# Constant-operand products on TensorE during the pooled attention, and last stores issued from two queues

## The reference, cut to what matters

```python
q_d = q.reshape(B, H, Sd, factor, D).mean(axis=3)      # factor = 4, Sd = 144; k_d, v_d likewise
out_up = np.repeat(sm_attn(q_d, k_d, v_d), factor, axis=2)
mask = np.abs(pos[:, None] - pos[None, :]) < factor
scores = np.where(mask, scale * np.matmul(q, k.transpose(0, 1, 3, 2)), -1000000000.0)
...                                                    # softmax, times v: out_local
x = out_up + out_local                                 # then (B * S, H * D)
xn = x / rms * rms_g;  g = xn @ w_gate;  silu = g * (1.0 / (1.0 + np.exp(-g)))
y = silu * (xn @ w_val) @ w_out
h = y @ w_in;  r = np.maximum(h, 0.0);  return (s * (r * r) + b) @ w_out2
```

## Time and profile before

| what | value |
|---|---|
| median of 3 runs | 991.49 us (990.32 to 991.92) |
| the profiled execution's own time | 987.57 us |
| its span, first to last instruction | 985.8 us |
| PE busy | 947.4 us, 96% |
| DVE busy | 547.3 us, 56% |
| ACT busy | 355.0 us, 36% |
| POOL busy | 372.5 us, 38% |

### The profile page before, as it was taken

One profiled execution on the slowest core, in us unless ns is written; L12 is line 12 of the kernel. 1 busy time (PEld: TensorE's weight loads), 2 busy tenths in 40 slices (PEclk: granted clock), 3 DMA queues, 4 the chain that ended last, 5 costly groups with the idle time before them and its releaser, 6 DMA issues.

```text
span 985.8 us, 12910 instructions
## 1 busy us (share of the span) xinstructions
PE 947.4 (96%) x4836; PEld 771.7 (78%) x4864; DVE 547.3 (56%) x818; ACT 355.0 (36%) x816; POOL 372.5 (38%) x192
## 2 busy tenths in 40 slices
PE   5698899999999999999999999999999999999997
PEld 4687799766777777777778998888888888888896
DVE  6899997875774765564542324434433443343343
ACT  3348854762324222422241444222222322222232
POOL 5757776777783876455600454000000000000000
PEclk9999999999999999999999999999999999999999
DMA  9797664433331231012003332102001100100010
GB/s 251 210 257 240 179 189 134 124 111 105 93 112 38 83 107 46 16 37 69 19 2 127 130 128 64 43 1 86 1 1 43 43 1 1 65 1 1 1 43 23
DMA packets 54379, 79.41 MB, mean 81 GB/s; under 512 B 9836, under 2 KB 37068, under 8 KB 52908
## 3 DMA queue, kind: packets, MB, share of 16 engines
q1 hardware_dynamic: 52444, 71.79, 24.6%
q10 hardware_dynamic: 1872, 6.78, 1.8%
HBM read 67.05 MB, written 11.50 MB: 80 GB/s over the span
## 4 chain that ended last, share of the span: by engine, by line
PE 82%; DVE 7%; DMA 4%; issue 2%; ACT 2%; SPq 1%; POOL 1%; DVEq 0%; ACTq 0%; POOLq 0%
PE bank L779 26%; PE bank L919 7%; PE bank L920 7%; PE bank L921 7%; PE bank L903 7%; PE bank L901 7%; PE bank L902 7%; PE bank L815 5%; PE bank L813 5%; PE bank L814 5%; DMA rawq<-in_q_dram 1%; DVE sc L594 1%; DMA rawv<-in_v_dram 1%; DVE x L604 1%; ACT prod_a L576 1%
## 5 line engine op out<-in xcount | busy, mean ns | idle before, releaser
L549 POOL TENSOR_TENSOR prod<-qs,ks 128x896 f32<-128x896 f32 x80 | 179.4, 2264 | 85.8 <-DVE sc L594 68.8
L563 POOL TENSOR_TENSOR prod<-sc,vs 128x896 f32<-128x896 f32 x72 | 138.1, 2020 | 65.5 <-DVE x L604 31.3
L940 DVE SCALAR_TENSOR_TENSOR r<-bank,r 128x512 f32<-128x512 f32 (+1 forms) x80 | 51.1, 638 | 181.0 <-ACT r L928 181.0
L903 PE MATMUL bank<-y_h,w2i_l 128*128 128x512 f32 (+1 forms) x320 | 117.7, 368 | 0.0
L928 ACT ACTIVATE r<-bank 128x512 f32<-128x512 f32 (+1 forms) x80 | 44.4, 555 | 181.9 <-PE bank L903 181.2
L835 DVE TENSOR_TENSOR bank<-bank,u 128x512 f32<-128x512 f32 (+1 forms) x66 | 39.5, 599 | 116.9 <-PE bank L779 116.3
L813 PE MATMUL bank<-h_h,wo_h 128*128 128x512 f32 (+1 forms) x264 | 102.7, 389 | 0.0
L779 PE MATMUL bank<-x_h,wv_h 128*128 128x512 f32 (+1 forms) x264 | 100.4, 392 | 0.0
L594 DVE TENSOR_REDUCE sc<-prod 128x14 f32<-128x896 f32 x80 | 85.7, 1077 | 17.0 <-POOL prod L549 16.9
L815 PE MATMUL bank<-h_h,wo_l 128*128 128x512 f32 (+1 forms) x264 | 93.3, 353 | 0.0
L814 PE MATMUL bank<-h_l,wo_h 128*128 128x512 f32 (+1 forms) x264 | 92.5, 350 | 0.0
(11 more groups left out here) (135 smaller groups left out, 1941.1 us busy)
## 6 DMA issues: line engine op xcount, KB each, us to landing
raww<-in_moe_w_out_dram SPq DMA_DIRECT2D x14, 512.0 KB, 4.3
ks<-in_k_dram SPq DMA_DIRECT2D x16, 280.0 KB
vs<-in_v_dram SPq DMA_DIRECT2D x16, 280.0 KB, 4.3
y_scr<-y_st ACTq DMA_DIRECT2D x4, 1024.0 KB, 4.1
raww<-in_moe_w_in_dram SPq DMA_DIRECT2D x8, 512.0 KB, 3.8
y_raw<-y_scr SPq DMA_DIRECT2D x4, 1024.0 KB, 4.8
out_dram<-o_st SPq DMA_DIRECT2D x16, 256.0 KB, 2.8
rawq<-in_q_dram SPq DMA_DIRECT2D x3, 1152.0 KB, 13.6
```

Source lines behind the costliest of these rows:

```text
L549: pool.tensor_tensor(dst, qv, kv, ALU.mult).then_inc(prod_ready, 1)
L563: pool.tensor_tensor(dst, pv, vv, ALU.mult).then_inc(prod_ready, 1)
L903: last = pe.matmul(o, w2i_l[:, m, kk, :], y_h[t % 2][:, kk, 0:w], start=False, stop=kk == DT - 1)
```

## The change

A bfloat16 tile `junk` is filled with ones by DVE, as its first instruction. PE multiplies the tile with itself, 128 x 128 by 128 x 512, into the bank of coarse scores that is about to be overwritten: 12 times before anything else, 2 times each behind the second and the fourth unit of transposes of batch 0, and 2 times in front of the coarse scores of heads 0 to 23, behind the wait for the exponents of head n-3 and ahead of the wait for the copied q and k. In all 64 products, whose results nobody reads. At the end PE raises a new semaphore `o_first` when the first of the two last results is complete, ACT copies that one on this signal, and the four stores are split: SP issues part 0 of each result, ACT part 1.

```diff
+                if r == TILES * M2 - 1 and tt == 0:
+                    last.then_inc(o_first, 1)
             last.then_inc(o_step, 1)
...
         def copy_out(eng, t, by_act):
-            eng.wait_ge(o_step, M2 * (t + 1))
+            if t == TILES - 1 and by_act:
+                eng.wait_ge(o_first, 1)
+            else:
+                eng.wait_ge(o_step, M2 * (t + 1))
...
+        def store_last(eng, tt, part):
+            eng.wait_ge(o_copied[tt], TILES)
+            eng.dma_start(out_l[2 * tt + part], o_st[part * LASTG:(part + 1) * LASTG, tt, :]).then_inc(o_stored[tt], 16)
...
-            for tt in range(2):
-                sp.wait_ge(o_copied[tt], TILES)
-                for part in range(2):
-                    sp.dma_start(out_l[2 * tt + part], ...).then_inc(o_stored[tt], 16)
+            store_last(sp, 0, 0)
+            store_last(sp, 1, 0)
...
             copy_out(act, TILES - 1, True)
+            store_last(act, 0, 1)
+            store_last(act, 1, 1)
...
+            dve.memset(junk[:, :], 1.0).then_inc(fill_made, 1)
             dve.memset(kT[D:JH, :, :], 0.0)
...
+            pe.wait_ge(fill_made, 1)
+
+            def keep_running(o, count):
+
+                for _ in range(count):
+                    pe.matmul(o[:, :], junk[:, 0:P], junk[:, :], start=True, stop=True)
+
+            keep_running(CSC[0], 12)
             pe.wait_ge(consts_made, 4)
             pe.wait_ge(pad_made, 1)
...
             for i in range(UNITS):
                 turn_pooled(0, i)
+                if i in (1, 3):
+                    keep_running(CSC[0], 2)
...
                     wait(pe, cexp, 2 * (n - 2))
+                    if n < 24:
+                        keep_running(CSC[n % 3], 2)
```

More of the change, by code:

```diff
@@ L293, in build @@
         HB, OB = [bank[0], bank[4], bank[1], bank[5]], YB
-        consts_made, pad_made = sem("consts_made"), sem("pad_made")
+        consts_made, pad_made, fill_made = sem("consts_made"), sem("pad_made"), sem("fill_made")
         small_loaded = sem("small_loaded")
@@ L333, in build @@
         h2_done, r_ready, sq2_done, g_ready, gh_ready, gl_ready = sem("h2_done"), sem("r_ready"), sem("sq2_done"), sem("g_ready"), sem("gh_ready"), sem("gl_ready")
-        o_step = sem("o_step")
+        o_step, o_first = sem("o_step"), sem("o_first")
         o_copied = [sem(f"o_copied{i}") for i in range(FAC)]
@@ L1127, in _ @@
                 store_out(sp, t)
-            for tt in range(2):
-                sp.wait_ge(o_copied[tt], TILES)
-                for part in range(2):
-                    sp.dma_start(out_l[2 * tt + part], o_st[part * LASTG:(part + 1) * LASTG, tt, :]).then_inc(o_stored[tt], 16)
+            store_last(sp, 0, 0)
+            store_last(sp, 1, 0)
             for tt in range(FAC):
```

## The result

The changed kernel takes 995.34 us in the median of 5 runs (993.26 to 997.67), the kernel before 990.32 us in its 5 (989.06 to 991.92). The ratio is 1.0047, with a 95% interval of 1.0028 to 1.0066: slower by 3 to 6.5 us. The forecast of 988.8 us was wrong in its direction; what happened is rival B, whose chance had been put at 0.22.

A forecast was written before the change was run, and what follows sets the result against it. DVE was taken to bound the first tiles, then x of tile 1, PE's work and the stores. Savings of 1.6 us from full clock and 1.1 us at the end, together 2.7, took 991.49 to 988.8 us; range 986.0 to 997.0.

The forecast's parts named there:

- rival B: At the heads, PE stays at half clock, each pair costs 1.0 us and DVE gets scores late: 997.2 us, chance 0.22.
- I take the full one for most of the stretch: At the heads with pairs, PE was to run at full clock, a step taking 1.8 us instead of 2.4.
- All that was to follow from full clock: Faster PE over the heads and first network was to bring x of tile 1 and the end 1.6 us earlier.
- Clock of the kernel before: From its first transposes to 130 us, PE was read as at half clock, despite the granted clock shown as 1.00.
- DVE sets the pace: In the first tiles DVE is the bound; a faster PE takes out little more than one 1.8 us wait.
- the 0.9 at head 8: DVE's 1.82 us wait at head 8 was to shrink by 0.9 us through faster transposes and scores.
- the 0.5 us for the gate at 165 us: A 0.56 us wait for the first network's gate was to go as PE reaches that network earlier: 0.5 us.
- The end: Earlier copy and stores split over two queues were to save 1.1 us, between 0.7 and 1.75.
- the DMA engines' 2.3 us: At the end, four stores keep the DMA engines busy for 2.3 us, ending no sooner than 983.9 us against 984.9.
- Front products: Twelve products ahead cost 0; the four among the first transposes cost 0 at full clock, 0.4 us at half.

The follow-up runs named there:

- e5: Changed kernel with six products instead of two in front of each of heads 0 to 23; 1.0061 of the kernel before.
- e7: Kernel before with the new stores, no constant products, and q and k in reduced float32 so coarse scores take one pass; 0.9984 of the kernel before.
- e6: Changed kernel without the pairs at the heads, with ten products in PE's pause ahead of head 8; 0.9968 of the kernel before.
- e1: Kernel before with only the new end and split stores, no fill and no constant products; 0.9991 of the kernel before.
- e3: Changed kernel without the 24 pairs in front of the heads, products at the front kept; 0.9973 of the kernel before.
- e12: Changed kernel with four products instead of two in front of each of heads 0 to 23; 1.0017 of the kernel before.
- e11: Kernel before with the new stores and only the ten products in PE's pause ahead of head 8; 0.9977 of the kernel before.
- e9: Changed kernel with the pairs in front of the heads 32 columns wide instead of 512; 1.0000 of the kernel before.

## Why the prediction was wrong, step by step

**The step that failed** is the one sentence "I take the full one for most of the stretch", with its reason that a pair comes every 3 us. Two products a head did not hold the clock: it was at half from 29 us, with each pair 0.86 us. All that was to follow from full clock, 1.6 us, fell away, and the lateness of rival B came in its place. I had measured the one piece of evidence that counts, 30 us of small products at half clock without a rise, and weighed it less than the hope in twelve dense ones at the start.

**Clock of the kernel before.** Right: read from pitches, against the column. The changed kernel's record shows both levels, and the same scores take 1.17 us at 0.50 and 0.66 at 1.00 (e5), which confirms that they had run at half.

**Rival B's sizes.** The mechanism is the one found, its price was too high. A pair costs 0.86, not 1.0 us: the switch after bfloat16 adds nothing here. Head 15 came 3.2 us late relative to the stage's start (forecast 3.6), head 20 4.4 (5.9), head 23 4.6 (6.8). By 0.86 the same working gives 7 x 0.86 - 3.24 - 0.14 = 2.6 for head 15, 4.2 for head 20 and 4.7 for head 23. So B should have said +3.5 and not +5.7 us.

**DVE sets the pace.** Right, and shown by e7 and e6: 18 us less PE work give 0.9 us, full clock at head 8 gives 0.8. It also holds behind the stage, where everything from L698 of tile 1 on takes the same 772 us in all profiles. So of the sum's 1.6 us the 0.9 at head 8 are there if the clock is up; the 0.5 us for the gate at 165 us were not tested.

**The end.** Forecast 1.1 us, measured 1.3 in twelve profiles with the new end (4.1 against 5.4). I had set the DMA engines' 2.3 us as the limit; in the changed kernel they are busy for 0.07 + 0.98 + 0.76 = 1.8 us, from 992 to 995 us. In time the gain of e1 alone is not settled.

**Front products.** Forecast at no cost: right, the stage of e3 is not longer, and e3 and e6 are the fastest kernels. What I missed is that even at full clock a product in front of the scores is on DVE's chain wherever PE was just released: at full clock I counted a step as 1.8 us of load and not as 0.56 us of delay. e5 and e12 show it.

**The best version** is e6: the new end and ten products in the one long pause of PE, 0.9968 (0.9954 to 0.9982) of the kernel before. e3 and e11 can't be told from it.

**Luck** is in every single profile. The two weight splits and the poolings took 2.4 to 6.6 us and 0.8 to 2.5 us by which of DVE and POOL started first, up to 4.1 us of one profile's time, as much as the effect that was looked for. Neither the sum nor a rival had a term for it. **Open** is whether products in front of the first heads move the stage's start, and with it why the time of e9 is above that of e3.

## What to carry to other kernels

Before filling an engine to keep its clock up, find out whose clock the stage hangs on: here PE was busy for 95% of a stretch and yet 18 us less work gave 0.9 us. If filling is wanted, put it in a pause that ends with a wait for something else, so that it ends before the release, and never between a release and the work that others wait for. And test whether the amount holds the clock in the trace; too little costs twice, once at half speed and once without the return. And before reading a few microseconds between two profiles, compare the durations of the same DVE instructions in both.

## What the runs showed of the hardware

In the kernel before, the granted clock is reported as 1.00 for the first 130 us, while the pitches show half speed; e1 and e7, without products, have the same, and the kernels with products at the front have both levels from 5 to 8 us on. In the kernel before, the first level that the trace records begins at 130.1 us, which is where the pitches change: ahead of the first record the column shows 1.00 whatever the clock, and the pitches are to be trusted.

Small float32 products of 72 x 72 and transposes, 95% busy for 30 us, left the clock at half. With two, four and six bfloat16 products of 512 columns a head, 3 to 4 us apart, the granted clock from 47 to 77 us was 0.50, 0.89 and 0.94. The Trainium skill ("TensorE: Matmul & The Clock Gate", Part 1) says that the clock is set by how busy the matrix engine has been of late. These rows agree for the dense products; the small ones, busy for 28.54 of 30 us, did not raise it here.

The transposes and the small float32 products do run twice as fast once the clock is up: three transposes take 0.49 us in e5 and 0.85 at half clock, each with the last one's way through the array. The clock also falls around PE's waits for x of tile 1: in the changed kernel the stretch from 219 to 231 us has 0.86, with PE busy for 9.61 of the 12 us.

```profile
219.00:231.00 12.00, 9.61 (x35) 5.95 (x34) 8.47 (x25) 5.45 (x10) 6.45 (x3) 0.86 0.14 38
```

A DVE instruction that adds or subtracts two SBUF tensors is held up by a POOL instruction that is already running: the pooling of k took 2.52 us where POOL's product had started 0.6 us earlier, and ended 0.6 us behind it; it took 0.76 us where it started 0.47 us ahead of the product. Timelines of the kernel before, then of the changed one:

```profile
57.69 2.51 POOL L549 TENSOR_TENSOR prod<-qs,ks 128x896 f32<-128x896 f32 x1 [3.47 <-DMA ks<-in_k_dram]
58.29 2.52 DVE L995 TENSOR_TENSOR kd<-rawk 128x576 f32<-128x576 f32 x1
...
62.29 0.76 DVE L1004 TENSOR_TENSOR kd<-rawk 128x576 f32<-128x576 f32 x1
62.76 2.23 POOL L549 TENSOR_TENSOR prod<-qs,ks 128x896 f32<-128x896 f32 x1 [5.17 <-DMA ks<-in_k_dram]
```
